# Fused attention, expert layers and a gated feed-forward on one core: VectorE's order in the paired stage, and gated tiles that stay in PSUM

## The reference

```python
# block-sparse attention: 2 batches, 8 heads, 768 positions, head_dim 64 -> x (1536, 512)
for e in range(4):                                   # experts, F = 1024
    h = np.maximum(x @ w1[e], 0.0)
    out += p[:, e:e + 1] * (h @ w2[e])
h = out @ w_in                                       # d_ff = 2048
g = h * (1.0 / (1.0 + np.exp(-1.702 * h)))
return g @ w_out
```

## Time and profile before

| | |
|---|---|
| median of 3 runs | 838.86 us |
| profiled execution | 837.27 us, span 835.4 us |
| TensorE busy | 801.8 us (96%) |
| VectorE busy | 589.1 us (71%) |
| ScalarE busy | 399.2 us (48%) |
| GpSimd busy | 589.5 us (71%) |
| mean granted TensorE clock | 0.994 |

### The profile page before, as it was taken

How to read it: one execution, slowest core, us unless ns; L and a number is a source line. 1 busy time by engine, 2 the same in 40 slices (tenths; PEclk the granted TensorE clock), 3 DMA queues, 4 the chain that set the end, 5 groups by cost and what they waited for, 6 DMA issues and landing times.

```text
span 835.4 us, 13926 instructions
## 1 busy us (share of the span) xinstructions
PE 801.8 (96%) x4894; PEld 780.1 (93%) x4894; DVE 589.1 (71%) x1194; ACT 399.2 (48%) x863; POOL 589.5 (71%) x406
## 2 busy tenths in 40 slices
PE   5889999999999999999999999999999999999996
PEld 4688999999999999999999999999999999998996
DVE  6888656666655666778779778655666666878776
ACT  4765554444454453433443443444565543644652
POOL 3687756656655798787787884876688771976883
PEclk9999999999999999999999999999999999999999
DMA  9969556484434545444434523444444552543502
GB/s 268 270 127 360 205 204 195 161 300 166 188 140 158 216 176 195 142 173 158 184 132 158 206 109 139 150 178 188 177 189 167 200 205 111 213 178 139 228 1 75
DMA packets 39956, 148.91 MB, mean 178 GB/s; under 512 B 16208, under 2 KB 17360, under 8 KB 36688
## 3 DMA queue, kind: packets, MB, share of 16 engines
q1 hardware_dynamic: 39888, 148.03, 49.6%
HBM read 100.81 MB, written 47.21 MB: 177 GB/s over the span
## 4 chain that ended last, share of the span: by engine, by line
PE 80%; DVE 6%; POOL 5%; issue 3%; SPq 2%; DMA 2%; ACT 1%; DVEq 0%; ACTq 0%; POOLq 0%
PE bank L1609 26%; PE bank L1611 25%; PE bank L1610 25%; PE bank L1564 2%; DMA k_win<-k_w 2%; DVE xa L1330 1%; PE bank L1601 1%; DVE xb_last_lo L1336 1%; PE bank L1575 1%; POOL wd_lo L798 1%; SPq L549 1%; DVE h_raw L1381 1%; DVE xb_first_lo L1336 1%; POOL wu_lo L719 1%; POOL wd_lo L731 1%
## 5 line engine op out<-in xcount | busy, mean ns | idle before, releaser
L1320 DVE TENSOR_TENSOR xa<-bank,xa 128x384 f32<-128x384 f32 x208 | 115.9, 557 | 136.1 <-PE bank L1611 133.3
L1609 PE MATMUL bank<-h_hi,wd_hi 128*128 128x384 f32 x448 | 150.7, 336 | 0.3 <-DVE xa L1318 0.2
L1611 PE MATMUL bank<-h_lo,wd_hi 128*128 128x384 f32 x448 | 150.0, 335 | 0.0
L1610 PE MATMUL bank<-h_hi,wd_lo 128*128 128x384 f32 x448 | 149.9, 335 | 0.0
L798 POOL TENSOR_TENSOR wd_lo<-stage,wd_hi 128x512 fp32r<-128x512 f32 x60 | 88.1, 1484 | 54.6 <-ACT wd_hi L1061 54.0
L731 POOL TENSOR_TENSOR wd_lo<-stage,wd_hi 128x1024 fp32r<-128x1024 f32 x27 | 65.2, 2413 | 84.3 <-ACT wd_hi L986 84.3
L1029 ACT ACTIVATE h_hi<-bank 128x384 fp32r<-128x384 f32 x112 | 55.0, 491 | 138.2 <-DVE bank L1376 114.9
L1013 ACT ACTIVATE snap<-bank 128x384 f32<-128x384 f32 x141 | 69.1, 490 | 106.0 <-PE bank L1611 105.2
L1609 PE MATMUL bank<-xb_other_hi,wu_hi 128*128 128x384 f32 x336 | 112.5, 335 | 0.2 <-ACT snap L1013 0.2
L1611 PE MATMUL bank<-xb_other_lo,wu_hi 128*128 128x384 f32 x336 | 112.4, 335 | 0.0
L1610 PE MATMUL bank<-xb_other_hi,wu_lo 128*128 128x384 f32 x336 | 112.3, 334 | 0.0
(11 more groups left out here) (121 smaller groups left out, 2061.1 us busy)
## 6 DMA issues: line engine op xcount, KB each, us to landing
stage<-weights SPq DMA_DIRECT2D x25, 1024.0 KB, 5.0
split<-wu_hi SPq DMA_DIRECT2D x24, 896.0 KB, 3.6
split<-wu_lo SPq DMA_DIRECT2D x24, 896.0 KB, 5.5
wu_hi<-split SPq DMA_DIRECT2D x23, 896.0 KB, 6.3
wu_lo<-split SPq DMA_DIRECT2D x23, 896.0 KB, 8.1
stage<-weights SPq DMA_DIRECT2D x23, 512.0 KB, 4.6
k_win<-k_w SPq DMA_DIRECT2D x8, 720.0 KB, 8.6
v_win<-v_w SPq DMA_DIRECT2D x8, 576.0 KB, 8.9
```

The lines of the kernel that those rows point to most:

```text
L1320: nc.vector.tensor_tensor(at, y_bank(g, t), at, ALU.add).then_inc(y_taken, 1)
L1609: nc.tensor.matmul(dst, w_h, a_h, start=first, stop=False, skip_group_check=True)
L1610: nc.tensor.matmul(dst, w_l, a_h, start=False, stop=False, skip_group_check=True)
L1611: return nc.tensor.matmul(dst, w_h, a_l, start=False, stop=last, skip_group_check=True)
```

## The change

Four things are changed, all of them in the paired steps. (1) `gate` writes back to the bank. ScalarE's new `copy_tile` brings the tile to `h_raw`, for GpSimd's sums alone; `high_tile` and `low_tile` read the bank; `tile_out` holds the bank until the copy and, for the six single tiles, the low part are done. GpSimd's first two sums wait for the copy. (2) VectorE's order: P2 d1 and P3 d0 go ahead of `low_sum` 2 and 3 in part, P6 d1 ahead of the gate of C22, P7 d0 and the gate of C21 on either side of `low_sum` 4, P4 d0 behind the gate of C12, P4 d1 at the head of the next odd step, and in the odd step P1 d1 behind the low part of C11, P5 d0 behind the gate of C22. At the end both P2 additions go ahead of `low_sum` 2, both P3 ahead of `low_sum` 3, both P6 ahead of `low_sum` 4. (3) TensorE's P6 waits for P1's addition (same bank) and no longer for P3's; VectorE's addition of P6 waits for that of P3 (same place in `xa`). (4) ScalarE's `high_held` of P1 goes ahead of `keep(g, 2)`.

```diff
+        def tiles(g, c):
+            return len(TILES_2) * pair_of(g) + TILES_2.index((g % 2, c)) + 1
+        def copied(g, c):
+            return 4 * (2 * pair_of(g) + g % 2) + READY[c]
         def tile_out(eng, g, c):
             if paired(g):
-                eng.wait_ge(gated_done, ready(g, c))
+                eng.wait_ge(raw_done, copied(g, c))
+                if (g % 2, c) in TILES_2:
+                    eng.wait_ge(blo_done, tiles(g, c))
...
                 if n == 1:
-                    pool.wait_ge(gated_done, ready(g, "C12"))
+                    pool.wait_ge(raw_done, copied(g, "C12"))
...
                 elif n == 2:
-                    pool.wait_ge(gated_done, ready(g + 1, "C12"))
+                    pool.wait_ge(raw_done, copied(g + 1, "C12"))
...
-                nc.scalar.activation(moved_tile(g, c)[0], hidden_raw(g, c), ACT.Copy).then_inc(bhi_done, 1)
+                nc.scalar.activation(moved_tile(g, c)[0], hidden(g, c), ACT.Copy).then_inc(bhi_done, 1)
+            def copy_tile(g, c):
+                act.wait_ge(gated_done, ready(g, c))
...
+                nc.scalar.activation(hidden_raw(g, c), hidden(g, c), ACT.Copy).then_inc(raw_done, 1)
...
                     keep(g, 1)
+                    copy_tile(g, "C11")
                     high_tile(g, "C11")
...
+                    copy_tile(g, "C22")
+                    copy_tile(g, "C21")
                     high_tile(g, "C21")
                     if ffn:
                         sigmoid(g, "C12")
                     high_tile(g, "C22")
+                    copy_tile(g, "C12")
                     high_tile(g, "C12")
...
+                if name == "P6":
+                    dve.wait_ge(y_taken, taken(g, "P3", d))
...
-                nc.vector.tensor_tensor(lo, hidden_raw(g, c), hi.bitcast(F32), ALU.subtract).then_inc(blo_done, 1)
+                nc.vector.tensor_tensor(lo, hidden(g, c), hi.bitcast(F32), ALU.subtract).then_inc(blo_done, 1)
...
                 elif second(g):
+                    if paired(g - 3):
+                        take_product(g - 3, "P4", 1)
...
                     low_sum(g - 1, 1)
+                    low_tile(g, "C11")
                     take_product(g - 1, "P1", 1 if g + 1 < STEPS else 0)
-                    low_tile(g, "C11")
                     add_c22(g)
-                    if g + 1 < STEPS:
-                        take_product(g - 1, "P5", 0)
-                    else:
-                        take_product(g - 1, "P1", 1)
                     gate(g, "C22")
+                    take_product(g - 1, "P5" if g + 1 < STEPS else "P1", 0 if g + 1 < STEPS else 1)
...
-                    take_product(g - 1, "P5", 1)
                     continue
                 elif paired(g - 1):
+                    take_product(g - 2, "P5", 1)
                     low_tile(g - 1, "C12")
...
                     gate(g, "C11")
+                    take_product(g - 2, "P2", 1)
                     low_sum(g - 2, 2)
-                    take_product(g - 2, "P2", 1)
                     take_product(g - 2, "P3", 0)
-                    low_sum(g - 2, 3)
...
+                    low_sum(g - 2, 3)
                     take_product(g - 2, "P3", 1)
                     take_product(g - 2, "P6", 0)
                     add_c22(g)
+                    take_product(g - 2, "P6", 1)
                     gate(g, "C22")
+                    take_product(g - 2, "P7", 0)
                     low_sum(g - 2, 4)
-                    take_product(g - 2, "P6", 1)
-                    take_product(g - 2, "P7", 0)
+                    gate(g, "C21")
...
                     add_c12(g)
+                    gate(g, "C12")
                     take_product(g - 2, "P4", 0)
-                    gate(g, "C12")
-                    take_product(g - 2, "P4", 1)
+                    if not paired(g):
+                        take_product(g - 2, "P4", 1)
...
-                    pe.wait_ge(y_taken, taken(g, {"P3": "P5", "P6": "P3", "P7": "P6", "P4": "P7"}[name], d))
+                    pe.wait_ge(y_taken, taken(g, {"P3": "P5", "P6": "P1", "P7": "P6", "P4": "P7"}[name], d))
```

More of the change, by code:

```diff
@@ L258, in attention_moe_ffn @@
         blo_done = sem("blo_done")
+        raw_done = sem("raw_done")
         tsum_done = sem("tsum_done")
@@ L1038, in high_tile @@
                     act.wait_ge(up_done, ups(g0 - 1))
-                nc.scalar.activation(moved_tile(g, c)[0], hidden_raw(g, c), ACT.Copy).then_inc(bhi_done, 1)
+                nc.scalar.activation(moved_tile(g, c)[0], hidden(g, c), ACT.Copy).then_inc(bhi_done, 1)
+            def copy_tile(g, c):
+                act.wait_ge(gated_done, ready(g, c))
+                q = pair_of(g)
+                if c[2] == "1":
+                    wait_count(act, blo_done if g % 2 == 0 else tlo_done, len(TILES_2) * q if g % 2 == 0 else 4 * q)
+                    wait_count(act, tsum_done, 4 * q)
+                elif g % 2 == 0:
+                    wait_count(act, tlo_done, 4 * q - 1)
+                else:
+                    wait_count(act, tsum_done, 4 * q)
+                if not paired(g - 2):
+                    act.wait_ge(y_done, takes(g - 1))
+                nc.scalar.activation(hidden_raw(g, c), hidden(g, c), ACT.Copy).then_inc(raw_done, 1)
             def high_sum(g, n):
@@ L1177, in _ @@
                     high_moved(ph, 6)
+                if paired(g):
+                    high_held(g, "P1")
                 keep(g, 2)
@@ L1182, in _ @@
                     sigmoid(g, "C22")
-                if not paired(g):
+                if paired(g):
+                    copy_tile(g, "C22")
+                else:
                     high_hidden(g, "C22")
@@ L1187, in _ @@
                 if paired(g):
+                    copy_tile(g, "C21")
                     high_tile(g, "C21")
-                    high_held(g, "P1")
                     high_held(g, "P5")
@@ L1370, in gate @@
                     dve.wait_ge(c_done, 3 * (g - 1) + {"C11": 1, "C22": 2, "C12": 3}[c])
-                gated = hidden_raw(g, c) if paired(g) else hidden(g, c)
                 if g < FFN0:
@@ L1375, in gate @@
                     half = int(c[2]) - 1
-                    nc.vector.scalar_tensor_tensor(gated, hidden(g, c), 0.0,
+                    nc.vector.scalar_tensor_tensor(hidden(g, c), hidden(g, c), 0.0,
                                                    p_bc[:, q % 2, tokens(half)],
@@ L1380, in gate @@
                     dve.wait_ge(sig_done, 4 * (g - FFN0) + n)
-                    nc.vector.tensor_tensor(gated, hidden(g, c), sig[:, n % 2, :], ALU.mult).then_inc(gated_done, 1)
+                    nc.vector.tensor_tensor(hidden(g, c), hidden(g, c), sig[:, n % 2, :], ALU.mult).then_inc(gated_done, 1)
             def low_hidden(g, c):
@@ L1483, in _ @@
                     add_c22(g)
+                    take_product(g - 2, "P6", 1)
                     gate(g, "C22")
+                    take_product(g - 2, "P7", 0)
                     low_sum(g - 2, 4)
-                    take_product(g - 2, "P6", 1)
-                    take_product(g - 2, "P7", 0)
+                    gate(g, "C21")
                     if not paired(g):
                         low_hidden(g, "C22")
-                    gate(g, "C21")
                     take_product(g - 2, "P7", 1)
@@ L1534, in _ @@
                     key_maxima(u)
+            take_product(STEPS - 2, "P5", 1)
             low_tile(STEPS - 1, "C12")
             take_product(STEPS - 2, "P2", 0)
+            take_product(STEPS - 2, "P2", 1)
             low_sum(STEPS - 2, 2)
-            take_product(STEPS - 2, "P2", 1)
-            low_sum(STEPS - 2, 3)
             take_product(STEPS - 2, "P3", 0)
             take_product(STEPS - 2, "P3", 1)
+            low_sum(STEPS - 2, 3)
+            take_product(STEPS - 2, "P6", 0)
+            take_product(STEPS - 2, "P6", 1)
             low_sum(STEPS - 2, 4)
-            for name, d in TAKES[IN_PAIR + 4:]:
+            for name, d in TAKES[IN_PAIR + 6:]:
                 take_product(STEPS - 2, name, d)
```

## The result

The changed kernel takes 824.31 us (median of 4 runs, 823.69 to 824.63), the kernel before beside it 838.4. The ratio is 0.9829, with a 95% interval of 0.9807 to 0.985. In five later runs on another chip the changed kernel took 824.38 us (ratio 0.9831, 0.9807 to 0.9854). The forecast was 822.3, with a range of 819 to 830.

What follows compares the result with a forecast made beforehand. TensorE, busy 801.8 of 835.4 us, bounds the kernel, so only its gaps give time. Phase 1 9.2, phase 3 4.2, end 3.2: 16.6 us off 837.27 gives 820.7, as a median 822.3; range 819 to 830.

Steps and rivals of the forecast that it cites:

- The sum: Time saved over the paired steps: phase 1 9.2, phase 3 4.2, the end 3.2, together 16.6 us.
- R5: Rival: the skill's PSUM overhead makes bank low parts dearer, 2 us less saved, 824.3 us; chance 0.02.
- Low parts from the bank: VectorE's 60 single low parts fall from 57.3 to 32.9 us, 0.549 each, by reading the bank.
- R2: Rival: the low part stays slow from the bank as well, 832.4 us; chance 0.04.
- Wait A: Down P2 d1 waits for P2 d0's addition: phase 1's 0.81 us a pair goes; phase 3's 1.09 goes in part.
- Copies and what is queued behind them: ScalarE's 80 copies, 39 us, delay GpSimd's sums 0.6 us; no TensorE wait taken, upper end 0.2 a pair.
- R1: Rival: new waits take part of the old ones' place, up to 9 us back, 827 to 831; chance 0.20.
- B: Down P6 d1 waits for P3 d1's addition, 0.57 us a pair; goes because P6 no longer waits for P3.
- C: Down P7 d1 waits for P6 d1's addition, 0.21 us a pair in phase 1, 0.40 in phase 3; goes.
- R4: Rival: no telling effect, the freed time is lost to GpSimd's 0.6 us later sums, 838 to 840; chance 0.06.
- The end: After the last pair, P6 d0's wait shrinks to 1.5 us idle, no clock fall expected; 3.2 us less.

Runs made afterwards that it cites:

- e3: Changed kernel, but VectorE's low part of a single tile reads ScalarE's copy in `h_raw` instead of the bank; 835.25 us.
- e4: Changed kernel, but ScalarE's copy of the even step's C11 and C21 waits only for GpSimd's first sum of the pair before; 821.88 us.
- e1: Changed kernel with VectorE's old order and P6 waiting for P3's addition again; gated tiles stay in banks, copies stay; 838.63 us.
- e8: Kernel before with one change: TensorE's P6 waits for P1's addition instead of P3's; 837.57 us beside 837.98.
- e7: e4 with every copy made twice, one after the other; 836.56 us.
- e5: Changed kernel with one wait put back: TensorE's P6 waits for P3's addition again; 828.38 us.

## Why the prediction was right

**The sum.** It said 16.6 us; the profiled spans differ by 13.2. By stretch: 7.4 for phase 3 and the end, measured 7.7; 9.2 for phase 1, measured 5.9; and 0.4 us more in front, where the kernels do not differ. The time came closer than the sum: the profiled run was forecast at 820.7 and took 824.39, 3.7 off, but the 1.6 us added for the median of the kernel before hid about half of that, for the changed kernel's profiled run lies at its median. That is luck. The time alone, 824.31, would also fit R5 (824.3); the rows have to decide.

**Low parts from the bank.** 0.549 us each were forecast, 0.555 (40) and 0.551 (20) measured, and e3 shows that it is the source. The Trainium skill's 125 ns of overhead on PSUM against 60 on SBUF ("Perfetto Trace Analysis", Optimizing Scalar/DVE Operations) would by an estimate have made them some 65 ns dearer. The rows show no such step: 0.55 us for an undisturbed one from SBUF, 551 and 555 ns from the bank. So R5 falls, and R2, which had the slow form stay, with it.

**Wait A** went in phase 1 by the narrow margin computed. In phase 3 about 0.3 is left, where 0.53 was forecast; what P4 d0's addition costs at down P1 d0 is 0.07, forecast 0.15. That makes 0.4 a pair instead of 0.68. Against it stands 0.4 us at the first pair's down P1 d0, for which the sum had no term, so that the 4.2 us of phase 3's pairs came out nearly right (4.6) by two misses that offset each other.

**Copies and what is queued behind them** is the step that failed. The copies were put at no wait of TensorE. I had the right chain (GpSimd's fourth sum, `high_sum` 4, `keep` 1, up P7 in slot 20) and wrote "I take no wait; the upper end gives 0.2 us a pair". It costs 0.40 (0.47 between starts), and with it 0.24 at down P7 d0, since the low part of C11, `low_sum` 3 and P6 d0's addition come late too. In five pairs that is 3.2 us, nearly all of the 3.4 by which the sum was too large. The fourth sum itself was not late: it ends at 448.16, 1.9 us ahead of where slot 20 would have begun without a wait (450.01), within the 1.3 to 2.4 of the forecast. What I had not read is the wait inside `copy_tile`, which puts the copy and the high part of C11 behind the fourth sum. e4 takes that wait away and gets 3.2 us back in phase 1's trace, which is then 9.1 us shorter than before, where the sum had 9.2. It was R1's mechanism, at a third of its upper price.

**B, C and P6.** Both went. But I had costed A, B and C as separate terms of a sum. e1 and e8 show that they are not: VectorE's queue sets the time of P6 d1's addition, and if only the earlier waits go, TensorE gets there earlier and waits there longer. The terms add up only because the change also moves the last of them. In e1 and e8 nothing is gained, as R4 has it, but not for R4's reason: e8 has no copies and no later sums.

**The end.** 3.2 us were forecast, 2.9 measured between P3 d0 and the end of the span. The idleness before P6 d0 is 0.85 us, where I had 1.5, and P7 d0 then waits 0.73 for P6 d0's addition behind `low_sum` 3. The clock does not fall there, as forecast: matmuls stay 0.17 to 0.18 us apart behind either wait, and the granted clock from 811 to 822 us is 1.00.

## What to carry to other kernels

Waits of one engine for another in a row are not terms to be added: take one away and see whether the next in the same queue grows by as much, and move the last one too. When a producer is rerouted through a busy engine's queue, read every wait of the new instruction, for what it waits for holds all that is queued behind it. And an operand moved to PSUM frees VectorE from GpSimd, but the copy that it then needs sits in the chain to the next products: one copy cost no wait in phase 1 once its own wait was short (e4), and a second one cost 0.86 us in each pair there (e7).

## What the runs showed of the hardware

**VectorE beside GpSimd.** A VectorE instruction with two SBUF inputs waited for the running GpSimd instruction to end, in every trace (1.92 us instead of 0.55 in e3). With one input in a bank it never did: 60 low parts at 549 to 555 ns. From 281 us on, the changed kernel's trace has 253 instructions of VectorE with an input in a bank that start beside a running GpSimd instruction, and all take 0.54 to 0.57 us; the 32 low parts of sums that do so all end 0.81 to 0.83 us behind the GpSimd instruction. Who starts first decides who pays. In the changed kernel, `low_sum` 2 and GpSimd's fourth sum, a pair of phase 1 and one of phase 3:

```profile
445.50 0.95 DVE L1382 TENSOR_TENSOR xb_first_lo<-t_raw,xb_first_hi 128x768 fp32r<-128x768 f32 x1
...
445.54 2.62 POOL L832 TENSOR_TENSOR h_raw<-h_raw,t_raw 128x768 f32<-128x768 f32 x1
...
753.36 2.14 DVE L1382 TENSOR_TENSOR xb_first_lo<-t_raw,xb_first_hi 128x768 fp32r<-128x768 f32 x1
...
752.84 1.84 POOL L832 TENSOR_TENSOR h_raw<-h_raw,t_raw 128x768 f32<-128x768 f32 x1
```

In the first VectorE is 0.04 us ahead and takes its usual 0.95, and GpSimd takes 0.8 longer. In the second GpSimd is ahead and takes its usual 1.84, and VectorE 1.2 longer. The Trainium skill ("SBUF — State Buffer", SBUF: two separate sides) calls this an exclusive lock for the whole instruction, taken by whoever comes first; the traces agree.

**TensorE's clock.** After an idle time of 3.18 us (before), 3.89 (e1) and 2.52 (e8) the matmuls went to 0.32 us apart, half speed, 1.2 GHz; the stages behind show a granted clock of 0.58, 0.51 and 0.66:

```profile
823.00:829.00 6.00, 5.66 (x18) 5.69 (x19) 2.64 (x5) 0.00 (x0) 0.00 (x0) 0.51 0.10 35
...
828.00:832.00 4.00, 4.00 (x17) 4.00 (x17) 1.12 (x2) 0.00 (x0) 0.00 (x0) 0.66 0.41 148
```

(e1, then e8). After 0.85 and 0.73 us in the changed kernel and 1.41 in e5 they stayed at 0.173 apart. So the three long waits cost more than their length, by 1.4 to 2.4 us: 8 to 15 matmuls at 0.32 instead of 0.173, and the slower restart.
